# A fused DeltaNet and MLP kernel on one core: Gram products of keys and queries in two banks, by strips of 32 key columns

## What is computed

```python
k_n = k / (np.linalg.norm(k, axis=-1, keepdims=True) + 1e-06)
for t in range(S):
    y[:, :, t] = np.einsum('bhd,bhde->bhe', q[:, :, t], state)
    v_old = np.einsum('bhde,bhd->bhe', state, kt)
    state = state + bt[:, :, :, None] * np.einsum('bhd,bhe->bhde', kt, vt - v_old)
...
x = attn_out  # (3072, 384)
h = (x @ w1) * (x @ w2) @ w3 @ w_out
# second block
h = h @ w_in
solu = h * softmax(h)
out = layer_norm(solu) * g_ln @ w_out
```

## Time and profile before

| | |
|---|---|
| median of 3 runs | 772.83 us (772.46 to 775.34) |
| the profiled execution, its own time | 774.38 us |
| its span, first to last instruction | 772.7 us |
| mean granted TensorE clock | 0.999 of full |
| attention with the weight blocks | about 0 to 447 us of the span |
| second MLP | 447 us to the end |

### The profile page before, as it was taken

How to read it: one execution, slowest core, us unless ns; L and a number is a source line. 1 busy time by engine, 2 the same in 40 slices (tenths; PEclk the granted TensorE clock), 3 DMA queues, 4 the chain that set the end, 5 groups by cost and what they waited for, 6 DMA issues and landing times.

```text
span 772.7 us, 21207 instructions
## 1 busy us (share of the span) xinstructions
PE 741.6 (96%) x9012; PEld 664.5 (86%) x9012; DVE 451.2 (58%) x759; ACT 339.5 (44%) x704; POOL 66.6 (9%) x97
## 2 busy tenths in 40 slices
PE   7998898999999999899999999999999999999997
PEld 6666698998899899899999988888899999999987
DVE  1974973984695498378522444442456666656663
ACT  5636326333534433544244434443444444444443
POOL 2333200110020020002000000000000001000000
PEclk9999999999999999999999999999999999999999
DMA  9980360153036035104111494540000000000001
GB/s 260 322 260 13 102 180 21 41 148 95 24 95 168 17 87 149 56 30 118 43 37 43 164 285 151 160 140 1 0 22 23 22 22 23 23 20 20 21 22 31
DMA packets 41898, 66.87 MB, mean 87 GB/s; under 512 B 4312, under 2 KB 26968, under 8 KB 41816
## 3 DMA queue, kind: packets, MB, share of 16 engines
q1 hardware_dynamic: 38648, 59.00, 26.3%
q10 hardware_dynamic: 3168, 6.65, 2.6%
HBM read 46.76 MB, written 18.87 MB: 85 GB/s over the span
## 4 chain that ended last, share of the span: by engine, by line
PE 80%; DVE 9%; ACT 6%; issue 4%; DMA 2%; DVEq 0%
PE ps L1472 19%; PE ps L542 13%; PE ps L506 13%; PE ps L519 12%; PE ps L1376 5%; PE ps L1485 4%; ACT gd L1196 3%; PE ps L1388 3%; PE ps L531 3%; DVE kqs L918 2%; PE ps L1430 2%; ACT a L1204 2%; PE ps L1441 2%; PE ps L1360 1%; PE ps L1405 1%
## 5 line engine op out<-in xcount | busy, mean ns | idle before, releaser
L1264 ACT COPY asb<-ps 128x256 f32<-128x256 f32 x96 | 35.7, 372 | 151.4 <-PE ps L1472 150.6
L1078 DVE TENSOR_TENSOR msb<-asb,ps 128x256 f32<-128x256 f32 x96 | 39.7, 414 | 71.2 <-ACT asb L1264 66.7
L918 DVE TENSOR_TENSOR kqs<-ps,mask 64x512 f32<-64x512 f32 x48 | 33.0, 687 | 73.3 <-ACT a L1204 72.8
L542 PE MATMUL ps<-woh,uth 128*128 128x384 f32 x192 | 64.8, 337 | 0.5 <-DVE utl L459 0.5
L542 PE MATMUL ps<-woh,utl 128*128 128x384 f32 x192 | 64.5, 336 | 0.0
L542 PE MATMUL ps<-wol,uth 128*128 128x384 f32 x192 | 64.3, 335 | 0.0
L1472 PE MATMUL ps<-xh,w1h 128*128 128x256 f32 x288 | 57.4, 308 | 6.2 <-DVE msb L1078 6.2
L459 DVE TENSOR_TENSOR utl<-ps,uth 128x512 fp32r<-128x512 f32 x48 | 31.1, 686 | 48.2 <-ACT uth L349 48.2
L335 ACT ACTIVATE e<-ps,stats 128x1024 f32<-128x1024 f32 x24 | 26.8, 1116 | 67.3 <-DVE stats L425 67.3
L506 PE MATMUL ps<-mh,w34h 128*128 128x512 f32 x144 | 56.0, 389 | 0.0
L506 PE MATMUL ps<-ml,w34h 128*128 128x512 f32 x144 | 56.0, 389 | 0.0
(11 more groups left out here) (157 smaller groups left out, 1621.1 us busy)
## 6 DMA issues: line engine op xcount, KB each, us to landing
m_dram<-msb SPq DMA_DIRECT2D x42, 256.0 KB, 2.1
mrest<-m_dram SPq DMA_DIRECT2D x36, 256.0 KB, 5.8
kqs<-in_kq SPq DMA_DIRECT2D x20, 256.0 KB, 7.0
kqs<-in_kq SPq DMA_DIRECT2D x24, 192.0 KB, 5.7
vs<-in_vtok SPq DMA_DIRECT2D x6, 768.0 KB, 10.2
ks<-in_ktok SPq DMA_DIRECT2D x5, 768.0 KB, 6.2
mfirst<-m_dram SPq DMA_DIRECT2D x12, 256.0 KB, 6.1
out<-wst SPq DMA_DIRECT2D x12, 192.0 KB
```

The source lines that it names most:

```text
L542: ins = pe.matmul(ob[s], xx[:, j, k, :], w[:, 4 * j + k, :], start=(j == 0 and k == 0 and p == 0), stop=(j == 1 and k == 3 and p == 2))
L918: ins = dve.tensor_tensor(kqs[r, par, tile, 1 + bb, :, :], bank[r], mask[r, tile % NP, :].unsqueeze(1).to_broadcast([C, H, C]), ALU.mult)
L1078: dve.tensor_tensor(msb[:, f // 2 % 2, f % 2, :], asb[:, f % 2, :], bbank[f % 2], ALU.mult).then_inc(product, 1)
L1264: act.copy(asb[:, f % 2, :], abank[f % 2]).then_inc(a_kept, 1)
```

## The change

- Keys and queries have their own buffers: `kt` (keys) and `z` (for each `bb`, masked product and queries stacked). The reversed order of halves is now in where the results are written and no longer in how keys and queries are laid out; so every second tile's output goes by one DMA too.
- A Gram is now two: `key_gram` and `query_gram`, each with one bank (2 or 3, by g). Each head and batch takes two matmuls with 32 key columns as weights, the second key matmul with 32 moving columns only; 32 instructions a Gram where one Gram of 16 did both. Weights of 48 rows x 32 columns are used in `k_state` too, 32 instructions a tile for 16.
- Since the first 32 columns of every bank row are now the diagonal block, one copy of 128 partitions replaces four of 32.
- Order: key Grams 0 and 1 together, then 2 and 3 in two later slots, the query Grams of tiles 0 and 1 ahead of the second solve of the first half, those of tiles 2 and 3 in the second half. VectorE masks two tiles after the transposition and two in the second half.

```diff
-        kqs = buf("kqs", [P, 2, TPG, 3, H, C])
+        kt = buf("kt", [P, 2, TPG, H, C])
+        z = buf("z", [P, 2, 2, TPG, H, C])
...
-        gbank = ps[:, 2:4, :].rearrange("p b (h c) -> p (b h) c", c=P)
+        gbank = [ps[:, 2 + j, :].rearrange("p (h c) -> p h c", c=C) for j in range(NP)]
...
-                    if g == 0:
-                        sp.dma_start(out_rows[0:2, bass.ds(C * chunk, C), :], osb[:, g, :]).then_inc(o_sent[g], 16)
-                    else:
-                        for bb in range(2):
-                            for half in range(2):
-                                at = 64 * bb + HB * (1 - half)
-                                sp.dma_start(out_rows[2 + bb, bass.ds(C * chunk + HB * half, HB), :],
-                                             osb[at:at + HB, g, :]).then_inc(o_sent[g], 16)
+                    sp.dma_start(out_rows[2 * g:2 * g + 2, bass.ds(C * chunk, C), :],
+                                 osb[:, g, :]).then_inc(o_sent[g], 16)
@@ vector, group @@
                 product_of(0, 0)
-                if ahead:
-                    keep_pt(n + 1, nxt, 0)
                 product_of(0, 1)
-                if ahead:
-                    keep_pt(n + 1, nxt, 1)
                 right_hand2(n, 0)
                 product_of(0, 2)
-                if ahead:
-                    keep_pt(n + 1, nxt, 2)
                 product_of(0, 3)
                 if ahead:
-                    keep_pt(n + 1, nxt, 3)
                     system_rows(n + 1)
+                    for g in range(NP):
+                        keep_pt(n + 1, nxt, g, gbank[g])
                 product_of(0, 4)
...
                 product_of(1, 0)
                 if ahead:
+                    keep_pt(n + 1, nxt, NP, gbank[0])
...
                 product_of(1, 2)
+                if ahead:
+                    keep_pt(n + 1, nxt, NP + 1, gbank[1])
@@ scalar @@
-                for bb in range(2):
-                    for half in range(2):
-                        rows = slice(64 * bb + HB * half, 64 * bb + HB * (half + 1))
-                        ins = act.copy(gd[rows, tile * H:(tile + 1) * H, :],
-                                       gbank[rows, :, HB * half:HB * (half + 1)])
-                ins.then_inc(gd_kept, 1)
+                act.copy(gd[:, tile * H:(tile + 1) * H, :], bank[:, :, 0:HB]).then_inc(gd_kept, 1)
@@ tensor @@
+            def key_gram(par, tile, bank):
+                for h in range(H):
+                    for half in range(2):
+                        for bb in range(2):
+                            r, at = state_rows(bb), HB * half
+                            ins = pe.matmul(bank[half_rows(bb, tile % NP, half), h, 0:C - at],
+                                            kt[r, par, tile, h, at:at + HB], kt[r, par, tile, h, at:C],
+                                            start=True, stop=True)
+                ins.then_inc(gram, 1)
+            def query_gram(par, tile, bank):
...
+                            ins = pe.matmul(bank[half_rows(bb, tile % NP, half), h, :],
+                                            kt[r, par, tile, h, at:at + HB], z[r, par, bb, tile, h, :],
+                                            start=True, stop=True)
+                ins.then_inc(p_gram, 1)
+            def next_key_gram(n, tile):
+                i = TPG * (n + 1) + tile
+                pe.wait_ge(kt_in[(n + 1) % 2][tile // 2], 32 * ((n + 2) // 2))
+                if tile >= NP:
+                    pe.wait_ge(gram_kept, i + 1 - NP)
+                elif n == 0:
+                    pe.wait_ge(pt_made, tile + 1)
+                else:
+                    pe.wait_ge(x_low, i - TPG - 1)
...
+            def next_query_gram(n, tile):
+                i = TPG * (n + 1) + tile
+                pe.wait_ge(q_in[(n + 1) % 2][tile // 2], 32 * ((n + 2) // 2))
+                if tile < NP:
+                    pe.wait_ge(gram_kept, i + 1 + NP)
+                else:
+                    pe.wait_ge(x_low, i + 1 - TPG - NP)
@@ k_state @@
                 for h in range(H):
-                    for bb in range(2):
-                        r = state_rows(bb)
-                        ins = pe.matmul(chain[g][u_rows(bb), hc(h)], kqs[r, par, tile, 0, h, :],
-                                        us[r, g, bb, hc(h)], start=True, stop=True)
+                    for half in range(2):
+                        for bb in range(2):
+                            r, at = state_rows(bb), HB * half
+                            ins = pe.matmul(chain[g][half_rows(bb, g, half), hc(h)], kt[r, par, tile, h, at:at + HB],
+                                            us[r, g, bb, hc(h)], start=True, stop=True)
@@ outputs @@
                 pe.wait_ge(u2_kept, q + 1)
+                pe.wait_ge(pt_made, TPG if n == 0 else q + 1)
@@ transpose_y @@
-                if tt == 0 and ahead:
-                    pe.wait_ge(gram_kept, TPG * (n + 2))
-                    pe.wait_ge(pt_made, TPG * (n + 2))
+                if ahead:
+                    pe.wait_ge(pt_made, q + TPG + 1)
```

More of the change, by code:

```diff
@@ L45, with deltanet_moe_kernel @@
                       defaults=(None, None, None))
[L48 removed]
+def deltanet_moe_kernel(nc, keys, queries, ktok, vtok, beta, w1, w2, w3t, wo1, win, wo2, gln, out):
     out_rows = out.rearrange("(b s) n -> b s n", b=B)
@@ L636, in flat, with pair @@
             return view.rearrange("p a h c -> p (a h c)").rearrange("p (c n) -> p c n", n=P)
-        w3s = [flat(kqs[:, 1, t, 0:2, :, :]) for t in range(TPG)]
+        def pair(view):
+            return view.rearrange("p t h c -> p (t h c)").rearrange("p (c n) -> p c n", n=P)
+        w3s = [pair(t[:, 2 * tt:2 * tt + 2]) for tt in range(2) for t in (kt[:, 1], z[:, 1, 0])]
         w3s += [flat(a21[:, 1, :, :, :]), w3raw[:, 0, :, :], w3raw[:, 1, :, :],
@@ L773, in load_kq @@
                 for bb in range(2):
[L774 to L777, removed]
+                    sp.dma_start(kt[state_rows(bb), n % 2, 2 * tt:2 * tt + 2, :, :],
+                                 keys[n, bb, :, tt]).then_inc(kt_in[n % 2][tt], 16)
+                for bb in range(2):
+                    sp.dma_start(z[loaded_rows(bb), n % 2, bb, 2 * tt:2 * tt + 2, :, :],
+                                 queries[n, bb, 0:D + 16 * bb, tt]).then_inc(q_in[n % 2][tt], 16)
             def load_k(n):
@@ L1187, in scale_first_v, with keep_diagonal @@
                 ins.then_inc(v_first, 1)
-            def keep_diagonal(n, tile, gbank):
+            def keep_diagonal(n, tile, bank):
                 act.wait_ge(gram, TPG * n + tile + 1)
@@ L1509, in group @@
                     if early and n > 0:
-                        grams(n + 1, 0)
+                        for tile in range(NP):
+                            next_key_gram(n, tile)
+                    if ahead and tt == 1:
+                        for tile in range(NP, TPG):
+                            next_query_gram(n, tile)
                     if tt == 0:
@@ L1583, in lay_out @@
     return {
-        "kq": np.pad(np.stack([columns(k), columns(q)], axis=5), [(0, 0), (0, 0), (0, 64 - D)] + [(0, 0)] * 4),
+        "keys": columns(k),
+        "queries": np.pad(columns(q), [(0, 0), (0, 0), (0, 64 - D)] + [(0, 0)] * 3),
         "ktok": tokens(k),
```

130 lines of the change are left out of this document (59 added, 71 removed).

## The result

| | before | changed |
|---|---|---|
| median, us | 774.09 (772.46 to 778.45, 4 runs) | 798.78 (795.19 to 799.98, 4 runs) |
| the profiled execution's own time | 774.38 | 797.81 |
| its span, us | 772.7 | 796.1 |
| mean granted TensorE clock | 0.999 | 0.973 |
| TensorE records (matmuls, weight loads) | 9012 each | 11892 each |

The changed kernel takes 1.0302 times the time of before, 95% interval 1.0245 to 1.0359: slower, and outside the range of the prediction. One execution in this document, one of e5's four, ran in a slower state of the chip (917 us at a granted clock of 0.749) and is left out of e5's median and ratio.

The account below looks back on a forecast made before the run. TensorE, busy 741.6 of 772.7 us, was taken as the bound; shorter waits and blocks summed to -20.5 us, forecasting 752.5 us. Its own range was 746 to 758 (chance 0.64); 746 to 764 held 8 in 10.

Parts of the forecast that it names:

- blocks that change their shape: TensorE's Grams and keys times state in 32-column strips: four matmuls a head overlap; +2.2 and -3.0 us.
- The waits for the masks: TensorE's 15 Gram waits for VectorE's masking all go: -13.3 us, and -1.0 for their cost beyond the profile rows.
- `msb`: Four weight-product waits, before the last weight block of groups 1 to 4's first halves, go: -2.4 us.
- The first group's `msb`: Two weight-product waits, 2.5 us, in the first group's second half shrink only a little, a masking pair being added: -0.5 us.
- `Keys times state`: With 32-column weights in four places a pair of tiles takes 1.73 us for 2.00: -3.0 us over 11 pairs.
- The Grams: Key and query Gram at 1.00 us each, 2.00 a tile for 1.89: +2.2 us over 20 tiles (ends -3.8, +5.0).
- The opening: Key and query Grams before the first solve, where any slower block shows in full: +0.3 us (ends -0.5 and +1.8).
- The last output: The last tile's output goes in one DMA instead of four, saving issues: -1.0 us (ends -1.3 and 0).
- Loads: 0: Input loads keep their DMA count and nearly their bytes, are issued a group ahead, nobody waits: 0 us.
- Strips take turns: Rival: in every Gram and keys times state, strips on the same rows do not overlap; +34, about 807 us; chance 0.09.
- VectorE's waits return: Rival: masking tiles 2 and 3 in second halves delays VectorE's products for weight blocks; 758 to 764 us; chance 0.20.
- Partial overlap: Rival: two fifths of the strips' overlap lost, +21 us, or waits only renamed; 765 to 780 us; chance 0.07.

Follow-up runs that it names:

- e5: The changed kernel with every tile's output in two DMAs, 64 rows of one batch each; 796.42 us, ratio 1.0264.
- e1: The changed kernel, its banks and order kept, with 64 key columns as weights everywhere and four diagonal copies a tile again; 770.48 us, ratio 0.9971.
- e8: e1 with outputs in two DMAs, `u1` copy between those of key Grams 0 and 1, first group's masking pair later, opening's query Grams spread; 758.93 us.
- e6: The changed kernel without loads of keys, queries and values for groups 2 to 5, which reuse earlier data; 782.83 us, ratio 1.0126.
- e7: The changed kernel with the opening's four query Grams spread over three pieces of w3 @ w_out; 796.84 us, ratio 1.0301.
- e10: e8 with the opening's four query Grams back in one piece; 760.79 us, ratio 0.9828.
- e9: e8 with every Gram and keys times state in 32-column strips again, with one diagonal copy a tile; 796.01 us, ratio 1.0265.

## Why the prediction was wrong

**The step that failed** is in "blocks that change their shape". Its sum priced a strip by the time in the array alone, and its lower bound took the 25 to 27 ns of a matmul in the solve as a pace that could go on for 64 instructions. It named as the unknown only "what sharing the rows costs". The supply of instructions had no term, and none of the rivals held it; its cost is the 34.0 us of gaps and most of the 14 us of lower clock above. Hints of it were there: 66 packets of 16 KB on q8, and a gap of 0.15 inside a solve block.

This step alone does not account for the whole distance. e1, which has no strips, is only 2 us below before, where -20.5 had been forecast. What takes up its gain are the output DMA (+3.7 where the sum had -1.0), the waits of the new order for `u1` (3.8) and for `msb` in the first group (2.8), 5.2 us of issue gaps that are left, and the gain in `keys times state`, which goes with the strips. e8, which mends the DMA and these waits, is 14 us below.

The Trainium skill, "Runtime: NRT & Kernel Launch", Instruction fetch mechanics, states that an engine's instructions arrive in blocks of 256 and that the next is fetched while the current one runs, "mostly hidden". The traces agree with the blocks and the fetching ahead; "mostly hidden" holds for the kernel before (0.15 us) and not for this one, where gaps reach 5.82 us.

**The waits for the masks**, -13.3 and -1.0: right. No key or query Gram waits for VectorE. **`msb`**, -2.4: right, the four are gone, in e1 too, where no long gaps could cover them. **`ysb` and `rr`**, -1.8: right.

**The first group's `msb`**, -0.5: wrong in size. In e1, where the gaps do not cover it, one wait there is 2.8 for the 2.5 of before. In e8, where the added masking pair stands behind the third product, it is 0.5: the pair cost more than the earlier start gave.

**`Keys times state`**, -3.0: right in sign, too small. A pair takes 1.50 and not 1.73, -5.5. **The Grams**, +2.2: 1.92 a tile and not 2.00, +0.6, right in sign and within the range. **The opening**, +0.3: its key Grams alone were 2.8 faster, and they began 1.9 us earlier, the wait for the first keys being 0.4 for 2.2, which the sum had at nothing; then the gaps of 4.13 and 5.82 came.

**The last output**, -1.0: wrong in sign, +3.7. I had reckoned the four issues saved and not what a DMA does whose outermost dimension is 2. At one to two tenths of the 16 engines, 192 KB took over 6 us, while two of 96 KB over 64 rows land in 2.1. The trace of before had shown it: its own one-DMA output, issued at 764.91 and of the same shape, trickled in the same way, until the four of 48 KB came (763 to 773):

```profile
DMA  0000000000000101120120111112717271600000
...
out<-wst SPq DMA_DIRECT2D x4, 48.0 KB, 1.7
```

The Trainium skill, "DMA: Bandwidth & Descriptors", "Why a DMA increments its semaphore by 16 and not by 1", says that the number of engines is the largest up to 16 that divides the slowest dimension of both sides, here 2. The rows of before, of the change and of e5 agree with it.

**"Loads: 0"** was wrong too. Their bytes are nearly the same, but they are in the way of the instructions: without those of groups 2 to 5 (e6) the ratio falls from 1.0302 to 1.0126.

**The rivals.** *Strips take turns* (807) came nearest in time and is refuted as a mechanism. A pair of key Grams took 1.81 us, where strips in turns would take 3.0 (16 heads at 188 ns), so two strips on shared rows overlap. That the time came near is chance. The rule of the Trainium skill ("TensorE: Matmul & The Clock Gate", Part 3), that a weight load overlaps only with another row group, is not what these blocks show. *VectorE's waits return*: one wait for `msb`, of 2.0, is left, at the end of the stage. *Partial overlap*: no; at 1.50 a pair `keys times state` is faster than the 1.73 that I had taken for full overlap.

## What to carry to other kernels

Count what an edit adds to an engine's instruction stream, and where. Here TensorE was never sent 256 instructions (matmuls and weight loads above all) more often than once in 3.3 us. In a stretch that runs through them faster, fewer and larger matmuls helped (e1, e8); moving small ones apart in the opening did not (e7, e10). An idle time that stands inside a block and has "issue" as its releaser is the sign to look for. Before the change is made, the records of the densest stretch, divided by its time, can be set against the 13 ns. And a saved DMA issue is worth nothing if the one DMA that is left runs on two engines: look at its outermost dimension.

## What the runs showed of the hardware that was not expected

- Two matmuls of 48 rows x 32 columns on the same rows and in different columns run at the same time as two on the other rows: 64 of `keys times state` take 1.50 us, 23 ns each, with a weight load for each.
- At the gaps of the changed kernel an instruction page's packet took 0.9 to 1.4 us, and TensorE went on 1.3 to 1.7 us after it had landed. With the DMA engines free it started 0.65 us after TensorE had entered the instruction page before; with all 16 busy (206 to 402 GB/s of loads), 3.2 to 5.4 us after, and gaps of 3 to 6 us arose.
- The granted clock fell to 1.2 GHz at or behind eight of the gaps of the changed kernel, of 1.4 to 5.8 us, and stayed there for 3.4 us or more, over work that was then mostly without gaps. In e9 this lasted 51.2 us in all; at the price of the block above that is 19 us beside the 26.8 of the gaps themselves.
- Gaps may not be independent: where one was made small (e7), another came. With the same instructions in the same order up to there, the gap at 52 to 53 us was 3.5 in e1 and 0.8 in e10. A clean estimate of one gap's worth could not be made.

What stays open: why the gap falls at instruction 193 to 195 by the trace's count and not at 0, which may be only where the trace begins to count; why a packet starts late behind loads, in the DMA queues or before them, which no run took apart; and why some gaps lower the clock and others do not.
